# Two tiles' tail keys turned by one transpose, scores by key ranges of 256 and 320, weight rounding in four pieces

## What is computed

```python
scores = q @ k.T / 8                       # per head, 576 x 576
thresh = max(scores, axis=-1) - tau
scores = where(scores >= thresh, scores, -1e9)
attn   = exp(scores - max) ; attn /= sum(attn) + 1e-9
x      = attn @ v                          # heads side by side: 2304 x 512
h = x @ w_in1 ; g = h * tanh(softplus(h)) ; x = g @ w_out1
h = x @ w_in2 ; g = h * clip(h + 3, 0, 6) / 6 ; out = g @ w_out2
```

## Time and profile before

| | |
|---|---|
| median of 3 runs | 1047.8 us (1047.51 to 1048.72) |
| profiled execution, its own time | 1048.76 us |
| its span | 1046.6 us, 19806 instructions |
| granted TensorE clock, mean | 1.00 |
| TensorE busy | 1024.9 us, 98% of the span |
| VectorE / ScalarE / GpSimd busy | 855.6 / 662.0 / 546.7 us |
| attention steps | from 7.7 us to about 320 us |
| rest of the last pairs' mixing between layer 1's first products | to about 340 us |

### The profile page before, as it was taken

One profiled execution on the slowest core, in us unless ns is written; L12 is line 12 of the kernel. 1 busy time (PEld: TensorE's weight loads), 2 busy tenths in 40 slices (PEclk: granted clock), 3 DMA queues, 4 the chain that ended last, 5 costly groups with the idle time before them and its releaser, 6 DMA issues.

```text
span 1046.6 us, 19806 instructions
## 1 busy us (share of the span) xinstructions
PE 1024.9 (98%) x6856; PEld 920.5 (88%) x6856; DVE 855.6 (82%) x1694; ACT 662.0 (63%) x1241; POOL 546.7 (52%) x562
## 2 busy tenths in 40 slices
PE   6999999999999999999999999999999999999998
PEld 5666666666666999999999999999999999999998
DVE  7877877877773889978997889967996779968884
ACT  6778777778885566555664566646564655655643
POOL 7787887888983770078204770087103760068200
PEclk9999999999999999999999999999999999999999
DMA  6364564564542799869895899742785448843674
GB/s 189 103 215 144 161 215 143 162 215 140 177 146 82 225 327 308 321 199 294 297 371 187 266 328 315 289 142 106 250 310 163 165 164 274 281 151 127 221 242 161
DMA packets 136034, 224.37 MB, mean 214 GB/s; under 512 B 9216, under 2 KB 76288, under 8 KB 135936
## 3 DMA queue, kind: packets, MB, share of 16 engines
q1 hardware_dynamic: 135936, 223.12, 64.4%
HBM read 172.49 MB, written 50.59 MB: 213 GB/s over the span
## 4 chain that ended last, share of the span: by engine, by line
PE 79%; DVE 8%; ACT 7%; issue 4%; DMA 1%; SPq 0%; DVEq 0%; ACTq 0%
PE banks L601 8%; PE banks L548 7%; PE banks L666 7%; PE banks L668 7%; PE banks L667 7%; PE banks L703 6%; PE banks L702 6%; PE banks L701 6%; PE banks L709 5%; PE banks L711 5%; PE banks L710 5%; PE banks L560 5%; PE banks L556 3%; ACT relu L870 3%; PE banks L581 2%
## 5 line engine op out<-in xcount | busy, mean ns | idle before, releaser
L1330 POOL TENSOR_TENSOR ring<-raw,ring 128x256 fp32r<-128x256 f32 x336 | 282.3, 874 | 379.5 <-ACT ring L835 379.5
L666 PE MATMUL banks<-x_high,ring 128*128 128x384 f32 x672 | 226.7, 337 | 1.5 <-ACT probsT L774 0.8
L668 PE MATMUL banks<-x_high,ring 128*128 128x384 f32 x672 | 224.8, 334 | 0.0
L667 PE MATMUL banks<-x_low,ring 128*128 128x384 f32 x672 | 224.6, 334 | 0.0
L1010 DVE TENSOR_REDUCE neg_max<-banks 128x1 f32<-128x576 f32 x144 | 108.0, 750 | 55.6 <-PE banks L548 55.2
L703 PE MATMUL banks<-ring,g_low 128*128 128x256 f32 x504 | 142.6, 283 | 0.0
L702 PE MATMUL banks<-ring,g_high 128*128 128x256 f32 x504 | 142.6, 283 | 0.0
L701 PE MATMUL banks<-ring,g_high 128*128 128x256 f32 x504 | 142.6, 283 | 0.0
L666 PEld LDWEIGHTS banks<-x_high,ring 128*128 128x128 f32 x672 | 126.1, 188 | 7.7 <-issue 4.9
L667 PEld LDWEIGHTS banks<-x_low,ring 128*128 128x128 f32 x672 | 126.2, 188 | 0.0
L668 PEld LDWEIGHTS banks<-x_high,ring 128*128 128x128 f32 x672 | 126.1, 188 | 0.0
(11 more groups left out here) (100 smaller groups left out, 2227.7 us busy)
## 6 DMA issues: line engine op xcount, KB each, us to landing
ring<-w_out_mix SPq DMA_DIRECT2D x168, 512.0 KB, 5.0
raw<-w_in_mix SPq DMA_DIRECT2D x48, 896.0 KB, 5.9
w_in_mix<-prep_in SPq DMA_DIRECT2D x18, 896.0 KB, 5.4
w_out_mix<-prep_high SPq DMA_DIRECT2D x16, 896.0 KB, 4.7
w_out_mix<-prep_low SPq DMA_DIRECT2D x16, 896.0 KB, 5.8
q_raw<-qT SPq DMA_DIRECT2D x64, 144.0 KB, 2.9
k_raw<-kT SPq DMA_DIRECT2D x64, 144.0 KB, 2.9
prep_in<-w_in SPq DMA_DIRECT2D x64, 128.0 KB, 3.3
```

What stands on the lines that cost most here:

```text
L666: nc.tensor.matmul(dst, w[:, 0, cols], high, start=(t == 0 and m < 4), stop=False, skip_group_check=True)
L667: nc.tensor.matmul(dst, w[:, 0, cols], low, start=False, stop=False, skip_group_check=True)
L668: mm = nc.tensor.matmul(dst, w[:, 1, cols], high, start=False, stop=(t == KH - 1), skip_group_check=True)
L1330: nc.gpsimd.tensor_tensor(ring_slot(slot)[:, 1, :], raw[q % 2][:, m, :], f32(ring_slot(slot)[:, 0, :]), ALU.subtract).then_inc(w_low_ready, 1)
```

## The change

1. A tile's scores are two key ranges of 256 and 320 keys, in place of 288 and 288 (`key_ranges`). In tiles of even i the first range is keys 320 to 575, then 0 to 319; in tiles of odd i keys 256 to 575, then 0 to 255. Within the bank pair they lie side by side, so the tail keys, now keys 256 to 319, are at the end of a tile of even i and at the start of one of odd i.
2. Tiles 2j and 2j+1 of a pair write their probabilities side by side, so both tails are adjacent, and one transpose turns both, in the odd tile (`turns_tail`). Tile 8 has its own. That is 5 tail transposes and `keep_tail` copies a pair in place of 9; each copy is 128 x 128 into a tile `tailT`.
3. The key tail's products take all 128 rows: the values of the 64 tail keys lie beside 64 rows of zeros (`values_tail`, lower or upper rows). They go by 128 queries: 4 products for u = 0 and 6 for u = 1 in place of 2 and 2. The spread sums' last 64 queries also use all rows. Values come by four DMAs in place of two, and GpSimd writes the zeros once at the start.
4. A weight unit is rounded in four pieces of 2, 2, 2 and 1 blocks: behind steps 15, 16 and 17 and behind step 1 of the next iteration. The rests are formed in four pieces too.
5. `weigh` waits for `main_turned` of one tile more, since there are two double buffers of probabilities in place of three single ones; `keep_main` takes over a wait of `keep_tail`.

```diff
+    def tails_turned(t):
+        return t // PAIR_TILES * TURNS + t % PAIR_TILES // 2
+    def turns_tail(i):
+        return tail_first(i) or i == PAIR_TILES - 1
+    def key_ranges(i):
+        return ((X_KEYS, SEQ), (0, X_KEYS)) if tail_first(i) else ((Y_KEYS, SEQ), (0, Y_KEYS))
...
-        PREP_PARTS = (slice(0, 4), slice(4, MIXES))
+        PREP_PARTS = (slice(0, 2), slice(2, 4), slice(4, 6), slice(6, MIXES))
...
-                sp.dma_start(values[P - TAIL:P, b, MAIN, :], src[MAIN * P:SEQ, :]).then_inc(v_loaded[b], 16)
+                for j, first in ((0, Y_KEYS), (MAIN // 2, 0)):
+                    rows = src[first:first + X_KEYS, :].rearrange("(t p) d -> p t d", p=P)
+                    sp.dma_start(values[:, b, j:j + MAIN // 2, :], rows).then_inc(v_loaded[b], 16)
+                sp.dma_start(values_tail[0:TAIL, b, LOWER, :], src[X_KEYS:Y_KEYS, :]).then_inc(v_loaded[b], 16)
+                sp.dma_start(values_tail[P - TAIL:P, b, UPPER, :], src[X_KEYS:Y_KEYS, :]).then_inc(v_loaded[b], 16)
...
-                        after(pe, tail_kept, t - 2)
+                        after(pe, tail_kept, tails_turned(max(t - 2, 0)))
...
-                nc.tensor.transpose(turned_tail[s % 3], probs[:, s % 3, SEQ - P:SEQ], ident[:, :]).then_inc(tail_turned, 1)
+                i, own = t % PAIR_TILES, probs_of(t)
+                if turns_tail(i):
+                    tail = probs[:, tails_turned(t) % 2, SEQ - TAIL:SEQ + TAIL] if tail_first(i) else own[:, SEQ - P:SEQ]
+                    nc.tensor.transpose(turned_tail[s % 3], tail, ident[:, :]).then_inc(tail_turned, 1)
...
+                        for c0 in range(PART_AT[u], PART_AT[u + 1], P):
+                            i = a * (MAIN + 1) + c0 // P if c0 < MAIN * P else MAIN
+                            first, n = (0, P) if i != MAIN else (TAIL * a, TAIL)
+                            rows = tail_rows(i)
+                            mm = nc.tensor.matmul(mixed[u][DH * a:DH * a + DH, c0 - PART_AT[u]:c0 - PART_AT[u] + n],
+                                                  values_tail[:, b, rows, DH * a:DH * a + DH],
+                                                  tailT[:, b, i // 2, first:first + n], start=False, stop=True, skip_group_check=True)
...
-                    if s == 16 and it < ITS - 1:
-                        round_prep(0, it, 0)
+                    if s in (15, 16, 17) and it < ITS - 1:
+                        round_prep(0, it, s - 15)
                     if s == 1 and it > 0:
-                        round_prep(0, it - 1, 1)
+                        round_prep(0, it - 1, 3)
```

More of the change, by code:

```diff
@@ L159, in attention_and_layers, with bank_pair, scores_at, scores_of @@
         banks = psum("banks", [P, 8, BANK])
-        scores = [banks[:, 2 * s:2 * s + 2, 0:HALF] for s in range(3)]
+        def bank_pair(s):
+            return banks[:, 2 * (s % 3):2 * (s % 3) + 2, :].rearrange("p b n -> p (b n)")
+        def scores_at(s):
+            first, last = key_ranges(s % PAIR_TILES)[0]
+            return BANK - (last - first)
+        def scores_of(s):
+            return bank_pair(s)[:, scores_at(s):scores_at(s) + SEQ]
+        def probs_of(t):
+            at = SEQ if tail_first(t % PAIR_TILES) else 0
+            return probs[:, tails_turned(t) % 2, at:at + SEQ]
         turned = banks[:, 6, :]
@@ L544, in score_tile @@
                     if half == 1:
-                        after(pe, tail_kept, t - 2)
+                        after(pe, tail_kept, tails_turned(max(t - 2, 0)))
+                    first, last = key_ranges(i)[half]
+                    begin = BANK if half else scores_at(s)
                     for n, (lhs, rhs) in enumerate(products):
-                        mm = nc.tensor.matmul(scores[s % 3][:, half, :], lhs, rhs[:, HALF * half:HALF * (half + 1)],
+                        mm = nc.tensor.matmul(bank_pair(s)[:, begin:begin + last - first], lhs, rhs[:, first:last],
                                               start=(n == 0), stop=(n == len(products) - 1))
@@ L745, in round_k, with keep_main @@
                 nc.scalar.copy(k_high[k][:, :], k_raw[k % 2][:, :]).then_inc(k_high_ready[k], 1)
-            def keep_main(t, s):
+            def keep_main(t, s, pair):
                 p, i = s // PAIR_TILES, s % PAIR_TILES
                 act.wait_ge(main_turned, t + 1)
+                if i == 0:
+                    after(act, mixed_ready, 2 * pair - 2)
                 if i == MAIN:
@@ L758, in keep_main, with keep_tail @@
                 nc.scalar.copy(dst, src).then_inc(main_kept, 1)
-            def keep_tail(t, s, pair):
+            def keep_tail(t, s):
                 p, i = s // PAIR_TILES, s % PAIR_TILES
[L763 to L774, removed]
+                if turns_tail(i):
+                    act.wait_ge(tail_turned, tails_turned(t) + 1)
+                    nc.scalar.copy(tailT[:, p, i // 2, :], turned_tail[s % 3]).then_inc(tail_kept, 1)
             rounds = {3: 2, 5: 3}
@@ L939, in _ @@
                     if unit < LATE_UNITS and part == 1:
-                        for half in range(2):
-                            round_prep(*late_unit(unit), half)
+                        for n in range(len(PREP_PARTS)):
+                            round_prep(*late_unit(unit), n)
                     for b in (B22, B11, B12):
@@ L991, in weigh @@
                 dve.wait_ge(thresh_ready, t + 1)
[L993 to L995 removed]
+                after(dve, main_turned, t - 1)
+                nc.vector.scalar_tensor_tensor(out=probs_of(t), in0=scores_of(s), scalar=thresh[:, s % 3:s % 3 + 1],
+                                               in1=exps[:, s % 2, :], op0=ALU.is_ge, op1=ALU.mult,
                                                accum_out=sums[:, s // PAIR_TILES, i:i + 1]).then_inc(probs_ready, 1)
```

84 lines of the change are left out of this document (48 added, 36 removed).

## The result

| | before | changed |
|---|---|---|
| median | 1047.72 us (1047.51 to 1048.72) | 1040.17 us (1039.75 to 1040.62) |
| profiled execution, its span | 1048.76, 1046.6 us | 1039.75, 1037.8 us |
| last tile's scores start | 317.8 us | 302.7 us |
| layer 1, from its second block of products to layer 2 | 339.7 to 684.9: 345.2 us | 324.7 to 675.7: 351.0 us |

The ratio is 0.9928 (0.9914 to 0.9942): 7.6 us faster, where 16.3 were forecast. It lies inside the range and in the direction forecast, with less than half of the gain. The two stretches part it: attention gained 15.1 us, layer 1 lost 5.7, and from layer 2 on the time moved by 0.4. Within layer 1 the three stretches of up products (L666 to L668 in the kernel before) grew by 1.3, 2.5 and 2.5 us, and the down products together are 0.5 shorter. The profiled pair differs by 9.0 us, since the profiled run of before was 1.0 above its median.

A forecast was written before the change was run, and what follows sets the result against it. Attention was taken to last as long as TensorE's own list of work plus stalls. Terms of -5.6 - 2.3 + 0.2 - 2.4 - 7.8 + 0.7 + 0.9 = -16.3 us gave 1031.5 us against the median, range 1025 to 1041.

The forecast's parts named there:

- The step that failed: Layers: 0.36 us more ScalarE time a unit was to cost nothing, that engine being busy 175 of 300 us.
- unchanged windows of the layers: Sign expected in the profile after: the layers' windows stay as they were; no size beyond that.
- the key tail for u = 1: Mixing products in step 1 of a pair: 0.70 us in place of 0.69, a loss of 0.2 us.
- The stalls: Scores waiting for `keep_tail` in steps 0 and 3: 7.8 us regained over seven iterations, 0.7 left over.
- transposes: Tail transposes on TensorE, four of nine a pair dropped: a gain of 5.6 us.
- u = 0 of the key tail: Mixing products on TensorE: 1.02 us in place of 1.16, 16 times, a gain of 2.3 us.
- spread sums: TensorE's sums for u = 1: 0.70 us in place of 0.85, a gain of 2.4 us.
- Scores: Key ranges of 256 and 320 columns cost the same a pair as two of 288; upper bound 3 us more.
- (1): Rival: short rounding pieces pile up on ScalarE in steps 15 to 17 and still stall; 1038.6 us, chance 0.13.
- (2): Rival: `keep_main` sets the pace, TensorE's gains return as waits; 1041.8 us if all, about 1040 if nearly all, chance 0.11.
- (3): Rival: key-tail pieces paced by their weight loads, 2.7 us a pair in place of about 1.0; 1058 us, chance 0.05.
- (4): Rival: no effect, as ScalarE waits over 2 us for GpSimd in step 15 every iteration; about 1048 us, chance 0.03.

The follow-up runs named there:

- e2: Changed kernel, with VectorE's rests of layer 1's units in two pieces and ScalarE's rounding still in four: 1033.97 us, ratio 0.9862.
- e1: Changed kernel, with units prepared in layer 1 rounded on ScalarE and their rests formed on VectorE in two pieces: 1035.0 us, ratio 0.9878.
- b2: Kernel before, with rounding and rests in four pieces within layer 1 only and nothing else of the change: 1053.64 us, ratio 1.0045.
- e8: Changed kernel, with layer 1's rounding in two pieces and its rests on VectorE in seven: 1044.46 us, ratio 0.996.
- e10: Changed kernel, with GpSimd writing zeros in place of the rests of layer 1's first weights, four pieces kept: 1033.12 us (one run).
- e3: Changed kernel, with the key tail's loops over heads and queries exchanged, so the two heads' products of one piece follow each other: 1038.75 us, ratio 0.9908.
- e7: Changed kernel, with rounding and rests in two pieces everywhere, behind steps 16 and 1 as before: 1035.21 us, ratio 0.9875.
- b1: Kernel before, with units rounded during attention in four pieces, those within layer 1 in two, every tile still turned by its own transpose: 1044.21 us, ratio 0.9957.

## Why the prediction was right and wrong

**The step that failed** is "In the layers one more ScalarE time of 0.36 a unit meets an engine busy 175 of 300 us: nothing". For ScalarE it holds (e2). But the rests of that unit go into four instructions too, and in layer 1 they are VectorE's, which is busy 267 of 300 us. I did not count them, and the sign that the prediction named, unchanged windows of the layers, did not hold: TensorE idles 1.84 us of 300 there in place of 0.36. The rests are 36 instructions in place of 18 and take 27 x 1.036 + 9 x 0.715 = 34.4 us in place of 24.5. Of the 9.9 us more, 2.7 are the instructions' own and 7.2 are waits beside GpSimd, about 0.54 for each instruction that meets its subtractions. The net loss of layer 1 is 5.7. Shown from four sides: undone (e1, e2), alone (b2), in more pieces still (e8), and with GpSimd's subtractions taken away (e10, and the pieces of the changed kernel that run without them). How the other 4.2 us were hidden was not followed.

**The mis-sized term** is the key tail for u = 1: "loss 0.2" was 0.28 us a pair in step 1, 4.5 in all. The error is not the price of a 64-column piece, which was the stated doubt: with the same pieces in another order e3 takes the forecast 0.70. It was to price the pieces by the spread sums, whose two column halves alternate in the list, while the new loops issue all pieces of one head and then all of the other. For u = 0 the same costs 0.05: 0.49 against 0.44.

**The stalls** went, as forecast: steps 0 and 3 lost 0.47 and 0.57 (of 0.78, less the 0.21 that the second pair's step 3 also lost), 7.3 us over seven iterations against 7.1. The cause that I gave was half right. The forecast joined two, shorter pieces and tiles of even i without `keep_tail`; the second does it alone but for 0.16 an iteration (e7), and the first does 0.6 of 1.0 without it (b1).

**The other terms** held, by step lengths of a pair: transposes 0.05 + 0.11 + 0.11 + 0.10, so 5.9 us against 5.6; u = 0 of the key tail 0.09, so 1.4 against 2.3; spread sums 0.21, so 3.4 against 2.4. The chain gives them only the forecast 0.15: my reading that a step lasts exactly the sum of its chain was not exact, since before, the second pair's step 3 took 2.14 where the sum is 2.07. Scores are unchanged, with 320 columns at 0.145 and 256 at 0.12, so that a pair of ranges costs the 0.53 of before. With the stalls less the u = 1 loss this makes 13.5. Step 11 of an iteration (i = 2 of its second pair) grew by 0.1. Stalls in iterations 6 and 7 which the prediction did not name shrank: in steps 10 and 12 the scores had waited for `keep_tail` behind roundings of x on ScalarE, 1.1 us in all, of which 0.1 stays, and in steps 2 and 11 the spread sums had waited for `x`, 0.8 us, of which 0.2 stays. Together attention came to 15.1 in this profile. That is near 16.3, but by errors of both signs, so its nearness is in part luck.

**The rivals.** (1) Stalls that stay: no. (2) `keep_main` as the pace: in step 2 the main transposes start 0.67 us after the spread sums, where the tail transpose started 0.59 after them, so the step gains 0.05 in place of 0.11. Listed waits for `keep_main` are 1.1 us in attention, five of the six in step 11. (3) Products paced by their loads: no; 20 records of a pair's tail took 1.46 us, 0.073 each, and twelve took 0.70 in e3, with loads of 137 ns each. (4) ScalarE waiting for GpSimd in step 15: 0.3 us from 40 to 318 us.

On the loads: the Trainium skill, "TensorE: Matmul & The Clock Gate", Part 3, has them overlap only where the row group differs. The twelve records in e3, at 0.058 us each with loads of 137 ns, are on the same rows, so here too the trace does not agree.

## What to carry to other kernels

When a loop's split is changed, list every engine that runs over that split, in every phase: a split that feeds one engine sooner multiplies another's instructions. Price an instruction by its neighbours in the list and on the other engines, not by its size alone; a row from another loop order is no price for yours. And where two changes could each remove a stall, take them apart before crediting the more visible one.

## What was not expected of the hardware

**VectorE pays per instruction beside GpSimd.** A subtraction of two SBUF operands on VectorE takes 0.15 us and 0.27 for each 256 words with GpSimd still (an estimate from 684 and 417 ns), and about 0.54 more when it meets GpSimd's subtractions, at 256, 512 and 768 words alike. Splitting repeats both. GpSimd's own mean hardly moved with the pieces, 874 ns before, 871 after, 855 in e8. The Trainium skill, "SBUF — State Buffer", section "Who interferes with whom", says that a VectorE instruction with two SBUF inputs contends with a GpSimd instruction that reads SBUF, and not with one that only writes it, and that the shared ports are an exclusive lock. The trace agrees: `L1149` takes 0.80 us in the mean beside subtractions and 0.55 beside the writes of e10. I had not weighed this rule in the prediction.

**The order of the column halves counts.** Six float32 products for u = 1 take 0.70 us when the two halves of the array alternate in the list and 0.97 when three of one half come before three of the other. For four products it is 0.44 against 0.49. In e3 the records of the two halves start in pairs at the same time; in the changed kernel those of the second half begin 0.27 us after the first ones, so the two overlap only in the middle.

**A freed engine shows the next wait at once.** TensorE's steps 1 and 10 got 0.27 us shorter in e3, and step 11 gave 0.3 back by a wait behind a VectorE instruction on 128 x 9 words that takes 0.65 us in the mean and 1.08 at that place.
